# A new order for the first half's chunks and attention steps in a fused three-layer kernel

## The reference

```
layer 1  per token t:  y = r (state + (u*k) v^T);  state = w*state + k v^T
layer 2  x = y in rows of 384; gate logits = x @ w_gate; the top 2 of 4 experts
         per expert e: q,k,v = x @ wq[e], wk[e], wv[e] (64 wide);
         causal softmax(q k^T / 8) v @ wo[e], weighted by its gate
layer 3  xk, xr = mixes of a token with the one before it;
         out = sigmoid(xr @ w_r) * (relu(xk @ w_k)^2 @ w_v)      (hidden 1024)
```

## Time and profile before

| | |
|---|---|
| time, median of 3 runs (lowest to highest) | 703.1 us (702.91 to 703.39) |
| the profiled execution | 703.36 us, of which its span is 701.6 us |
| mean granted TensorE clock | 0.995 of full speed |
| TensorE busy | 683.9 us, 97% of the span |
| VectorE, ScalarE, GpSimd busy | 385.7 (55%), 320.9 (46%), 153.7 (22%) |
| chain that ended last | TensorE 93%, VectorE 3%, ScalarE 1%, GpSimd 1%, issue 1% |
| HBM read and written | 37.84 MB, 4.72 MB |

### The profile page before, as it was taken

How to read it: one execution, slowest core, us unless ns; L and a number is a source line. 1 busy time by engine, 2 the same in 40 slices (tenths; PEclk the granted TensorE clock), 3 DMA queues, 4 the chain that set the end, 5 groups by cost and what they waited for, 6 DMA issues and landing times.

```text
span 701.6 us, 12410 instructions
## 1 busy us (share of the span) xinstructions
PE 683.9 (97%) x4864; PEld 448.6 (64%) x4864; DVE 385.7 (55%) x753; ACT 320.9 (46%) x805; POOL 153.7 (22%) x199
## 2 busy tenths in 40 slices
PE   7969999999999999999999999999999999999998
PEld 7856666666656665666656665666665666566554
DVE  7897986382854656537463738637476223551200
ACT  2454566522662266622655227662175314563340
POOL 7772530053201601017010522004320000000000
PEclk9998999999999999999999999999999999999999
DMA  9996500004400080000800044000000000000000
GB/s 230 298 348 182 171 14 1 1 1 127 140 1 1 24 242 2 1 1 24 242 2 1 1 119 147 2 1 1 35 1 2 1 23 12 1 1 12 23 0 35
DMA packets 36922, 43.37 MB, mean 62 GB/s; under 512 B 2560, under 2 KB 27264, under 8 KB 36608
## 3 DMA queue, kind: packets, MB, share of 16 engines
q1 hardware_dynamic: 36864, 42.57, 20.8%
HBM read 37.84 MB, written 4.72 MB: 61 GB/s over the span
## 4 chain that ended last, share of the span: by engine, by line
PE 93%; DVE 3%; ACT 1%; POOL 1%; issue 1%; DVEq 0%; POOLq 0%; ACTq 0%
PE bank L924 81%; PE bank L928 6%; PE bank L1087 3%; PE bank L1083 3%; DVE idec L652 1%; DVE att L713 0%; ACT k_sb L442 0%; ACT shared L460 0%; DVE nmax L680 0%; DVE shared L693 0%; POOL rk_sb L345 0%; ACT shared L451 0%; DVE dec L644 0%; DVE cmp L761 0%; POOL rk_sb L343 0%
## 5 line engine op out<-in xcount | busy, mean ns | idle before, releaser
L924 PE MATMUL bank<-wv_sb,k_sb 128*128 128x384 f32 x384 | 139.4, 497 | 0.0
L924 PE MATMUL bank<-xk_sb,wk_sb 128*128 128x384 f32 x384 | 138.1, 499 | 0.0
L924 PEld LDWEIGHTS bank<-xk_sb,wk_sb 128*128 128x128 f32 x384 | 68.4, 190 | 42.9 <-issue 5.5
L924 PEld LDWEIGHTS bank<-wv_sb,k_sb 128*128 128x128 f32 x384 | 67.5, 190 | 38.8 <-issue 3.7
L652 DVE RECIPROCAL idec<-dec 112x260 f32<-112x260 f32 x48 | 82.8, 1755 | 0.5
L451 ACT ACTIVATE shared<-bank,nmax 128x128 f32<-128x128 f32 (+5 forms) x96 | 59.9, 629 | 47.3 <-DVE nmax L680 47.3
L680 DVE TENSOR_REDUCE nmax<-bank 128x1 f32<-128x128 f32 (+5 forms) x96 | 55.4, 619 | 46.7 <-PE bank L924 46.7
L376 POOL TENSOR_TENSOR state<-state,carry 112x512 f32<-112x512 f32 x20 | 22.0, 1099 | 260.1 <-DVE state L732 133.4
L924 PE MATMUL bank<-xT_sb,wqk_sb 128*128 128x384 f32 (+1 forms) x240 | 64.1, 424 | 0.6 <-ACT xT_sb L498 0.6
L481 ACT ACTIVATE att<-ident,bonus 128x128 f32<-128x128 f32 x192 | 58.0, 391 | 13.7 <-DVE bonus L660 10.7
L673 DVE TENSOR_TENSOR out_sb<-bank,sg_sb 128x384 f32<-128x384 f32 x24 | 13.4, 557 | 85.2 <-PE bank L924 84.9
(11 more groups left out here) (91 smaller groups left out, 922.2 us busy)
## 6 DMA issues: line engine op xcount, KB each, us to landing
rk_sb<-in_rk SPq DMA_DIRECT2D x24, 384.0 KB, 7.1
v_sb<-in_v SPq DMA_DIRECT2D x24, 256.0 KB, 7.5
w_sb<-in_wT SPq DMA_DIRECT2D x24, 227.5 KB, 4.8
r_sb<-in_rT SPq DMA_DIRECT2D x24, 224.0 KB, 5.1
k_sb<-in_kT SPq DMA_DIRECT2D x24, 224.0 KB, 6.3
out<-out_sb SPq DMA_DIRECT2D x24, 192.0 KB, 1.9
wk_sb<-in_w_k SPq DMA_DIRECT2D x1, 1536.0 KB, 12.3
wv_sb<-in_w_v SPq DMA_DIRECT2D x1, 1536.0 KB, 16.1
```

The source lines that it names most:

```text
L924: return nc.tensor.matmul(out, lhsT, rhs, start=start, stop=stop)
```

## The change

Nothing that is computed changes, and no engine gets other work: four fewer dummy products are run, two loads change places, and calls change places in the lists of TensorE, ScalarE and VectorE. `diagonal(4)` and `diagonal(5)` are issued as two halves of four heads each; the waits stand ahead of the first half, and the semaphore is raised by the second. GpSimd's list stays.

```diff
-WARM_UP = 36
+WARM_UP = 32
@@ SyncE
             load_rk(0)
+            load_r_k(0)
             load_w(1)
-            load_r_k(0)
@@ ScalarE
-            def diagonal(n):
-                act.wait_ge(bonus_ready, n + 1)
-                if n >= 2:
-                    act.wait_ge(y_psum, n - 1)
-                for x in range(H):
+            def diagonal(n, half=None):
+                if half != 1:
+                    act.wait_ge(bonus_ready, n + 1)
+                    if n >= 2:
+                        act.wait_ge(y_psum, n - 1)
+                for x in range(H // 2 if half == 1 else 0, H // 2 if half == 0 else H):
...
-                i.then_inc(diag_ready, 1)
+                if half != 0:
+                    i.then_inc(diag_ready, 1)
@@ ScalarE
             keys_by_token(2)
-            diagonal(4)
             gate_exponentials(0)
             exponentials(0, 0)
             keys_by_token(3)
+            keys_by_token(4)
+            transposed(0, 0)
             exponentials(0, 1)
-            transposed(0, 0)
-            keys_by_token(4)
+            first_output(0)
             exponentials(0, 2)
             transposed(0, 1)
-            first_output(0)
-            diagonal(5)
+            diagonal(4, 0)
             exponentials(0, 3)
+            diagonal(4, 1)
             transposed(0, 2)
             first_output(1)
-            x_chunk(3)
             exponentials(0, 4)
             transposed(0, 3)
+            x_chunk(3)
+            diagonal(5, 0)
+            exponentials(0, 5)
             first_output(2)
+            transposed(0, 4)
+            diagonal(5, 1)
             x_chunk(4)
-            exponentials(0, 5)
-            transposed(0, 4)
             first_output(3)
+            transposed(0, 5)
+            first_output(4)
             x_chunk(5)
-            first_output(4)
-            transposed(0, 5)
             first_output(5)
@@ VectorE
-            dve.wait_ge(const_ready, 1)
             scan(0)
...
             inverse(1, 1)
+            dve.wait_ge(const_ready, 1)
             masks(0)
@@ VectorE
             inverse(5, 1)
+            inverse(5, 0)
             gate_weights(0, 0)
             maxima(0, 0)
-            inverse(5, 0)
+            gate_weights(0, 1)
+            scale(0, 0)
             state_update(2)
-            gate_weights(0, 1)
             maxima(0, 1)
-            scale(0, 0)
             masks(3)
             scale(0, 1)
             maxima(0, 2)
             state_update(3)
-            bonuses(5)
             scale(0, 2)
             maxima(0, 3)
+            bonuses(5)
+            scale(0, 3)
+            maxima(0, 4)
             masks(4)
-            scale(0, 3)
             state_update(4)
-            maxima(0, 4)
-            masks(5)
             scale(0, 4)
             maxima(0, 5)
+            masks(5)
             scale(0, 5)
@@ TensorE
             first_projections(0)
+            linear_scores(2)
             x_chunk(1)
-            linear_scores(2)
             first_projections(1)
@@ TensorE
             keys_by_token(4)
+            transposes(0, 0)
+            output(0, 0)
             update(3)
-            transposes(0, 0)
             score_step(0, 2)
+            linear_scores(4)
             transposes(0, 1)
-            output(0, 0)
-            x_chunk(3)
             score_step(0, 3)
             transposes(0, 2)
             output(0, 1)
-            linear_scores(4)
-            update(4)
+            x_chunk(3)
             score_step(0, 4)
             transposes(0, 3)
+            update(4)
+            linear_scores(5)
+            score_step(0, 5)
             output(0, 2)
-            linear_scores(5)
+            transposes(0, 4)
             x_chunk(4)
-            score_step(0, 5)
-            transposes(0, 4)
             output(0, 3)
+            transposes(0, 5)
+            output(0, 4)
             x_chunk(5)
-            output(0, 4)
-            transposes(0, 5)
             output(0, 5)
```

## The result

The changed kernel takes 708.56 us (median of 11 runs, 706.61 to 709.59), the kernel before on the same chips 703.42 (703.1 in the three runs shown ahead of the prediction). The ratio is 1.0069, with a 95% interval of 1.0058 to 1.008: slower, by some 5 us. The profiled execution took 709.31 us, its span 707.6. One execution of the first kernel of experiment 6 took 1156.55 us at a mean granted clock of 0.559 and is left out of its median and ratio.

A forecast was written before the change was run, and what follows sets the result against it. Bound: the head before experts_sum(0) at 76.3 us, the only place with idle TensorE time, paced by VectorE, then hand-overs. Order +0.6 and clock +2.7 = +3.3 on 703.36: 706.7, median 706.4 us; range 703.2 to 708.8.

The forecast's parts named there:

- closed loop: Tail: output(0, 3), transposed(0, 4), diagonal(5, 1), masks(5), scale(0, 5), transposes(0, 5) wait on one another, from 67.5 to 72.1 us.
- The gap: TensorE ahead of transposes(0, 5): idle for 4.6 us, from 67.5 to 72.1.
- Part 2, gates to `scale(0, 2)`: VectorE's new order: gates' first part 3.3 us, then 8.8, so scale(0, 2) ends at 54.5 us instead of 57.2.
- start of the gates: VectorE, behind bonuses and both inverses: the gates start at 42.4 us (42.0 to 42.8), before at 41.91.
- `scale(0, 2)` is held up by `carried(3)`: VectorE against GpSimd on the shared port pair: scale(0, 2) takes 1.6 us rather than 1.1.
- Part 3, the tail: Up to experts_sum(0): the 4 us lead is given back, experts_sum(0) starts at 76.9 us against 76.31.
- the clock's term: TensorE behind the late idle stretch: half clock for 6.8 us, costing 2.7 us (1.7 if half as long).
- (b) the clock falls early too: Rival, TensorE's waits behind the gates: half clock at about 50 us costs about 2.3 more, 708.7 us; chance 0.10.
- my likeliest case: Whole kernel with the late fall of the clock: 706.7 us profiled, 706.4 median; chance 0.58.
- It can't keep that: Ahead of the gates: VectorE, some 2.2 us ahead, loses this because products(4) needs a load; gates start at 42.4.
- can't start before 35.97: GpSimd's products(4): its load is issued at 28.97 us and takes 7.0, so it starts no earlier.
- The order alone costs 0.6 us: Head, clock's loss left out: experts_sum(0) starts at 76.9 us against 76.31 by the new order of calls.

The follow-up runs named there:

- first kernel of experiment 6: Changed kernel with its tail put back near the order before and 7 dummy products in the waits behind the gates: 700.37 us against 703.46 (4 runs).
- experiments 1 and 2: Changed kernel with one edit each: scale(0, 5) ahead of masks(5) on VectorE, 704.53 us; halves of diagonal(5) either side of exponentials(0, 4) on ScalarE, 703.09 us.
- early dummies: Changed kernel with 5 dummy products ahead of score_step(0, 1) and 2 ahead of transposes(0, 0): alone 707.25 us against 703.40.
- both sets of dummies: Changed kernel with dummy products behind the gates (5 and 2) and 16 in the gap ahead of transposes(0, 5): 704.55 us, ratio 1.0018.
- experiment 3: Changed kernel with dummy products in TensorE's waits: ahead of transposes(0, 5) 706.14 us, behind the gates 707.25, in both places 704.55.
- experiment 1: Changed kernel with scale(0, 5) ahead of masks(5) on VectorE: 704.53 us against 703.40, ratio 1.0014.
- experiment 4: Kernel before with dummy products in its waits behind the gates, 5 ahead of score_step(0, 1) and 9 ahead of transposes(0, 0): 701.15 us against 703.46.
- late dummies: Changed kernel with 16 dummy products between output(0, 3) and transposes(0, 5): 706.14 us against 703.40, ratio 1.0042.
- experiment 2: Changed kernel with the halves of diagonal(5) moved to either side of exponentials(0, 4) on ScalarE: 703.09 us against 703.46, ratio 0.9986.

## Why the prediction was right, and where it was not

**Direction and place: right.** Slower was given 0.65, the loss lies ahead of `experts_sum(0)`, and experiments 1 and 2, each cutting another link, show that the closed loop is its main cause. The gap was forecast as 4.6 us and is 4.69.

**Part 2, gates to `scale(0, 2)`: right at full clock.** From the start of the gates to `x_chunk(3)` I had 13.1 us (42.4 to 55.5); both profiles with the early dummies show 13.0. The gates' first part took 2.5 us (43.09 to 45.59) where I took 3.3; in the profile with both sets of dummies it took 3.1 (43.62 to 46.69). That `scale(0, 2)` is held up by `carried(3)` shows too: its wide pair takes 1.16 us in the changed kernel, against 0.73 in the kernel before, where it runs after `carried(3)` has ended. The price was of the right kind for the wrong reason in part: the small operation slipped in ahead of GpSimd, and the wide ones met it.

```profile
55.34 0.17 DVE L692 TENSOR_SCALAR rinv<-rsum 128x2 f32<-128x2 f32 x1
...
55.74 1.16 DVE L697 TENSOR_SCALAR shared<-shared,rinv,gate 128x256 f32<-128x256 f32 x2
```

By the Trainium skill (SBUF — State Buffer, "SBUF: two separate sides") the loser of the port pair "fully blocks"; the trace agrees for the wide pair, by 0.4 us here, while the reciprocal at 55.54, in the middle of `carried(3)` as well (55.38 to 56.43), took its usual 0.17 us.

**Part 3, the tail: right.** From `x_chunk(3)` to `experts_sum(0)` I had 21.4 us; the kernel at full clock takes 21.9 (56.67 to 78.58).

**The step that failed: the clock's term.** The text put +2.7 us on a late fall and took the early stretch of rows 2 for gone; "(b) the clock falls early too" had a chance of 0.10. The profile has both falls. The early one comes at 48.3 us already, lasts 10 us instead of 6.8 and costs 2.9 (experiment 3), against the 2.3 of rival (b). The late one costs 1.4 us (1.54 and 1.55 us where 0.84 and 0.88 are taken at full clock, in experiment 1), against my 2.7. My argument against (b) was that both waits are shorter than the one before. They are: 1.49 and 0.69 us. The clock fell all the same, and earlier. So rival (b) is what happened in the profiled execution, and its 708.7 is close to the measured median. The runs differ, though: the three at a mean granted clock of 0.995 took 706.6 to 707.0 us, near my likeliest case, the five at 0.99, the profiled one among them, 708.6 to 709.6. The profiled execution was forecast at 706.7 and took 709.3. That this sum was only 2.6 us short is in part luck, as its errors offset each other: the late fall 1.3 us too much, the early one 2.9 too little, the start of the gates 0.7 and part 3 0.5 too little. (A stretch of 6.8 us that begins up to 1.5 us before the work leaves at least 5.3 us of it, not 5.4, which changes nothing.)

**A second step that failed: "It can't keep that".** In the changed kernel `products(4)` does wait for its load, for 0.64 us, but I took this for the end of the matter. The length of the gates' first part and the waits of TensorE behind them still change, and that part of the change is worth 1.6 us. In the kernel before, `products(4)` began at 36.76 right behind GpSimd's own work, so there the load was not what held it. The gates began at 43.09, not 42.4. In the ten profiles where `products(4)` waits for the load, it begins anywhere between 34.6 and 37.9 us. So "can't start before 35.97" does not hold from run to run, and a term that hangs on that load is good to some 1.5 us either way in a single profile.

```profile
36.37 1.00 POOL L343 TENSOR_TENSOR rk_sb<-rk_sb 128x384 f32<-128x384 f32 x1 [0.64 <-DMA rk_sb<-in_rk]
```

**"The order alone costs 0.6 us"** compared my pass at full clock with a kernel before that had lost 2.3 us to its clock. The arithmetic holds (+0.6 against 76.31), but as a price of the order it is 3.4 us, all of it the loop's (experiment 4).

## What to carry to other kernels

When calls are moved in lists written by hand, follow each single-buffered hand-over round all engines once: a wait that is put behind another engine's late work closes a loop, and no list by itself shows it. Where two orders are compared, compare them at the same clock: a few dummy products in the waits of both kernels do it, and say what the clock alone is worth. A change ahead of a stage whose start does not move can still pay, here 1.6 us.

## What the runs showed of the hardware that I had not expected

TensorE's clock fell at 48.3 us, in the second of two waits of 1.49 and 0.69 us with 1.1 us of work between them, although it had held in the kernel before through 1.57 and 0.74 us and fell there only after 2.65 us more. The rows of the kernel before:

```profile
45.97 0.49 PE L924 MATMUL bank<-qk_sb 64*128 64x128 f32 x4 [1.57 <-ACT shared L451]
...
47.81 1.10 PE L924 MATMUL bank<-v_sb,ktok 128*112 128x128 f32 x8 [0.74 <-DVE state L734]
51.56 0.44 PE L928 MATMUL bank<-ident,shared 128*128 128x128 f32 x2 [2.65 <-DVE shared L693]
```

and of the changed one, round the fall (the row at 48.56 between them stands in the section on the result):

```profile
46.77 0.49 PE L928 MATMUL bank<-qk_sb 64*128 64x128 f32 x4 [1.49 <-ACT shared L451]
...
49.70 0.70 PE L928 MATMUL bank<-shared,val 128*64 128x128 f32 x4 [0.46 <-ACT shared L460]
```

In the profile of the late dummies it fell at 46.4 us, 0.3 us behind a single wait of 1.49. So short waits can be enough, and the longest single wait is not what to judge by. The Trainium skill (TensorE: Matmul & The Clock Gate, "A second HAM failure mode: psum-queue depth-cycling") tells of short idle spells between groups of matmuls, there from cycling through PSUM banks, that make the clock go back and forth; this trace agrees in kind, with other causes of the waits. How long such a stretch lasts was different too: 3.4, 6.8, 10.2 or 13.7 us in these profiles, and in the changed kernel TensorE was busy for 9.14 of 9.60 us of it.

A kernel's time then depends on it from run to run. In the kernel of experiment 2 the runs with a mean granted clock of 0.999 or 1.0 took 699.5 to 700.4 us (5 runs), those with 0.99 took 704.7 to 705.8 (3 runs), and the four between them 702.4 to 704.4.
